# Attention, experts and MLP on one core: the stores of the attention's rows issued by ACT instead of SyncE

## The reference, cut to what matters

```python
# attention: batch 4, heads 8, sequence 576, head size 64
scores = scale * q @ k.T                     # heads 0-3: the last 32 positions; heads 4-7: every 32nd
attn = exp(scores - max); attn /= attn.sum() + 1e-09
x = (attn @ v)                               # -> rows of 2304 tokens x 512
# experts: gate by x @ w_gate (8 experts), rows with x @ w_skip <= 0 pass through
out[sel] = x[sel] + gate * (relu(x[sel] @ w1[e]) @ w2[e])
# then an MLP 512 -> 2048 -> 512 with leaky relu over all rows
```

## Time and profile before

| What | Value |
|---|---|
| median of 3 runs | 760.3 us (759.5 to 762.51) |
| the profiled execution's own time | 757.96 us |
| its span in the trace | 755.9 us |
| busy, of the span | PE 712.7 us (94%), DVE 279.1 (37%), ACT 231.7 (31%), POOL 184.3 (24%) |
| chain that ended last, by engine | PE 86%, DVE 4%, DMA 3%, ACT 3%, issue 3% |
| attention | from the start to the end of the last `xo`, 139.8 us |
| stores `x_rows<-xo`, local (8) | 288.0 KB each, median 7.5 us from issue to landing |

### The profile page before, as it was taken

How to read it: one execution, slowest core, us unless ns; L and a number is a source line. 1 busy time by engine, 2 the same in 40 slices (tenths; PEclk the granted TensorE clock), 3 DMA queues, 4 the chain that set the end, 5 groups by cost and what they waited for, 6 DMA issues and landing times.

```text
span 755.9 us, 12260 instructions
## 1 busy us (share of the span) xinstructions
PE 712.7 (94%) x4674; PEld 662.7 (88%) x4674; DVE 279.1 (37%) x597; ACT 231.7 (31%) x505; POOL 184.3 (24%) x173
## 2 busy tenths in 40 slices
PE   4999999776998999999999999999999999999997
PEld 3899999666998999998999998999999899999996
DVE  5867778458212111113232223223232322323222
ACT  2667666331111111122232223222232322223222
POOL 5242220104197777761100300210030011001000
PEclk9999999896999999999999999999999999999999
DMA  8484845574788989940100200110020001001001
GB/s 174 107 190 114 230 123 158 171 251 124 275 266 285 307 286 310 316 151 20 42 1 1 84 1 0 43 42 1 0 83 0 0 28 55 0 0 43 1 0 42
DMA packets 68653, 81.76 MB, mean 108 GB/s; under 512 B 26137, under 2 KB 47417, under 8 KB 68602
## 3 DMA queue, kind: packets, MB, share of 16 engines
q1 hardware_dynamic: 60040, 58.60, 26.0%
q0 software_dynamic: 7504, 22.44, 9.3%
q10 hardware_dynamic: 1058, 0.02, 0.1%
HBM read 68.84 MB, written 12.21 MB: 107 GB/s over the span
## 4 chain that ended last, share of the span: by engine, by line
PE 86%; DVE 4%; DMA 3%; ACT 3%; issue 3%; SPq 0%; another core or an unknown queue 0%; POOL 0%; ACTq 0%; POOLq 0%; DVEq 0%
PE psum L1679 26%; PE psum L1696 26%; PE psum L1565 9%; PE psum L1581 8%; PE psum L1443 4%; PE psum L1464 3%; ACT kt L884 2%; PE psum L1415 2%; PE psum L1453 2%; PE psum L1434 1%; PE psum L1598 1%; PE psum L1591 1%; DVE sc L1063 1%; DMA x_sb<-x_rows 1%; DMA x_rows<-xo 1%
## 5 line engine op out<-in xcount | busy, mean ns | idle before, releaser
L1380 DVE SCALAR_TENSOR_TENSOR g_act<-g_raw 128x384 f32<-128x384 f32 x96 | 53.6, 558 | 229.4 <-ACT g_raw L1019 229.4
L1679 PE MATMUL psum<-x2h,wih 128*128 128x384 f32 x384 | 130.7, 340 | 1.5 <-issue 1.5
L1679 PE MATMUL psum<-x2h,wil 128*128 128x384 f32 x384 | 129.4, 337 | 0.0
L1679 PE MATMUL psum<-x2l,wih 128*128 128x384 f32 x384 | 128.9, 336 | 0.0
L1019 ACT ACTIVATE g_raw<-psum 128x384 f32<-128x384 f32 x96 | 47.2, 492 | 235.7 <-PE psum L1679 235.7
L1696 PE MATMUL psum<-woh,g_l 128*128 128x512 f32 x288 | 114.0, 396 | 0.0
L1696 PE MATMUL psum<-wol,g_h 128*128 128x512 f32 x288 | 113.7, 395 | 0.0
L1696 PE MATMUL psum<-woh,g_h 128*128 128x512 f32 x288 | 112.2, 390 | 0.5 <-DVE g_l L1384 0.5
L857 POOL DMA_INDIRECT out_dram<-o_sb,idxo x15 | 16.0, 1067 | 282.7 <-ACT o_sb L1014 279.7
L1565 PE MATMUL psum<-xt,wring 128*128 128x160 f32 x512 | 81.6, 305 | 1.5 <-issue 1.5
L1581 PE MATMUL psum<-hp,wring 128*128 128x160 f32 x512 | 78.4, 299 | 1.3 <-issue 0.7
(11 more groups left out here) (210 smaller groups left out, 869.0 us busy)
## 6 DMA issues: line engine op xcount, KB each, us to landing
wring<-in_moe_w_dram SPq DMA_DIRECT2D x64, 512.0 KB
x_sb<-x_rows SPq DMA_DIRECT2D x4, 1024.0 KB, 6.3
stage<-in_moe_w_in_dram POOLq DMA_DIRECT2D x4, 1024.0 KB
stage<-in_moe_w_out_dram POOLq DMA_DIRECT2D x4, 1024.0 KB
q_st<-in_q_dram SPq DMA_DIRECT2D x7, 576.0 KB
k_st<-in_k_dram SPq DMA_DIRECT2D x7, 576.0 KB
vs<-in_v_dram SPq DMA_DIRECT2D x20, 128.0 KB, 8.2
x_rows<-xo SPq DMA_DIRECT2D x8, 288.0 KB, 7.5
```

The lines of the kernel that those rows point to most:

```text
L1380: dve.scalar_tensor_tensor(out=g_act[:, f % 2, :], in0=g_raw[:, f % 2, :], scalar=LEAK, in1=g_raw[:, f % 2, :], op0=ALU.mult, op1=ALU.max) ...
L1679: last = pe.matmul(bank[f % 2][:, 0:MT * P], wt[:, c, f * P:(f + 1) * P], xp[:, T.par, c, :], start=(c == 0 and n == 0), stop=(c == KD - 1 ...
```

## The change

The stores leave SP's list. ACT issues each of them after the exponentials of the group four places on, and the last four after its last `probs_out`. The wait for `s_xo` moves with them. Nothing is computed otherwise, and the DMAs are the same in number, shape and address.

```diff
@@ SP @@
                     sp.wait_ge(s_xo, NG * b + g + 1)
-                    if g in (2, 5) or g >= NL:
-                        x_store(sp, b, g)
                     if b + 1 < B:
                         v_load(sp, b + 1, g)
@@ ACT @@
+            def stored(b, g):
+                if g in (2, 5) or g >= NL:
+                    act.wait_ge(s_xo, NG * b + g + 1)
+                    x_store(act, b, g)
+
...
                     exps(b, g)
+                    if NG * b + g >= 4:
+                        stored(*divmod(NG * b + g - 4, NG))
...
             for g in (NG - 2, NG - 1):
                 probs_out(B - 1, g)
+            for g in range(NG - 4, NG):
+                stored(B - 1, g)
```

## The result

The changed kernel takes 752.16 us (median of 6 runs, 751.3 to 755.44), the kernel before, run beside it, 759.9 us (6 runs, 757.51 to 762.51). The ratio is 0.9909, with a 95% interval of 0.9885 to 0.9934: faster by 0.9%. (Of 759.9 us that is 6.9 us; the two medians by themselves lie 7.7 apart, in six runs each that spread over 4 to 5 us.) The forecast was 755.8 us with a range of 753.3 to 763.0; the time lies 1.1 us under that range. The direction and the mechanism came as forecast; the gain is larger than the sum said. The profiled execution took 751.3 us, with a span of 749.5 (before: 757.96 and 755.9).

The account below looks back on a forecast made before the run. PE was taken to wait at the attention's end for loads of v that SP issues late; -4.6 + 1.1 - 0.3 - 0.7 = -4.5 us, from the 760.3 us median to 755.8 us, range 753.3 to 763.0.

Parts of the forecast that it names:

- What bounds the kernel now: Attention's end, batch 3: PE waits ahead of the last two values products for loads of v that SP issues late.
- the loads of v aren't the cause: Rival: both gaps at the attention's end stay, only ACT's costs remain: +1.1 us, 761.4 us; chance 0.05.
- The end of the attention: Last values products: both gaps go, last xo at 135.2 instead of 139.8 us: -4.6 us, bounds -5.1 and -4.2.
- The stores leave SP: SP's list: 21 stores, 13.8 us, go; last loads of v issued until about 122.4 instead of 136.2 us.
- The stores on ACT inside the pipeline: Three boundaries between batches: stores on ACT delay copies of k that PE awaits: +1.1 us, bounds 0 and +4.8.
- The start of the router: After the last xo: clock stays up, but ACT's stores and zero row come late: -0.3 us, bounds -0.7 and +0.9.
- The last data: Router's fourteenth tile: last store goes out earlier, PE's wait for x_load(3) goes: -0.7 us, bounds -0.7 and 0.
- ACT's stores queue behind SP's issues: Rival: each store on ACT waits half an SP issue, 0.4 us: sum -0.4, 759.9 us; chance 0.19.
- ACT inherits SP's long stalls: Rival: stalls like SP's 2.75 and 3.48 us hit ACT's stores, 4.3 us per boundary: 768.7 us; chance 0.14.
- ACT hides all of it: Rival: no cost at the boundaries and the clock's full gain: -6.5 us, some 754 us; chance 0.10.

Follow-up runs that it names:

- The pair with the delay: 28 unread transposes added to PE's list in batch 0 of both kernels: the kernel before 756.87 us (1.0005), the changed kernel 753.29 us (0.9957).
- SP with its list filled up again: The changed kernel with 21 filler DMAs on SP where stores of batches 0 to 2 had stood: 763.54 us, 1.0087 against the kernel before.

## Why the prediction was wrong in size

*What bounds the kernel now* was right: the gaps are waits for loads that SP issues too late. The pair with the delay shows that SP's list sets the end, and SP with its list filled up again brings the gap back. The rival "the loads of v aren't the cause" falls.

*The end of the attention* is the step that failed, as a term of the sum that was sized too small: "**-4.6 us**", with bounds of -5.1 and -4.2. With the boundaries it said -3.5 us for the last `xo`; the means over three executions say 134.78 - 140.04 = -5.3. Nearly all of the difference of 1.8 us lies in three parts, all readable. I had taken PE's position from one execution, where it reached batch 1 at 45.75; the changed kernel's mean is 44.96: 0.8 us. I had taken SP's from the same one, with the last `xo` at 139.39, where the mean is 140.04: 0.65 us. And the boundaries cost 0.26 us less than the 1.1. My end for PE was good: from 139.39 - 3.5 = 135.9, less 0.8 and 0.26, comes 134.8, which is the measured mean. What failed is that this term is a difference between two chains, PE's and SP's list, and one execution gives one draw of it. The waits of the three executions of before show the same: 4.8 us in the one I used, 7.7 and 5.6 in the others. My bounds held only what the store on ACT could cost, not that the base could move.

*The stores leave SP*: the loads were to be issued by 122.4; it was 127.52, 125.11 and 126.22, in none of the three before 125. The 13.8 us took each store at its usual length and let the excess pass on, and it did pass. But SP's other DMAs grew by more than that excess: 88.5 - 76.6 = 11.9 us against 5.8 (9.4 us in the means of three executions). The sum held the rest of SP's list for fixed. It was without effect here, since the margin was large.

*The stores on ACT inside the pipeline*: "**+1.1 us**" against 3 x 0.28 = 0.84 measured. The mechanism is right to the hundredth at step 1 (0.81 us between the exponential and the copy of k); at step 9 I had allowed 0.05, and there was nothing. The store put ahead of the exponentials takes the whole away, which shows that this is the cost. At the attention's end the copy came 0.50 us later where I had +0.46.

*The start of the router*: "**-0.3 us**" against 0.0 (3.38 us in both kernels). "The clock should stay up" was wrong: it was at its lower level for 3.4 us instead of 6.8 (from windows of the kernel before: 0.59, 0.50, 0.50 and 0.70 between 136 and 144 us). In the other executions, read in the same way, it was 6.8 and 3.4 us in the changed kernel, and 10.2 us in the two others of the kernel before. What I had named as the counterweight, ACT's stores and the zero row, is the bound: with the clock held at 1.00 only 0.17 us are won, with the zero row away as well 0.68.

*The last data*: "**-0.7 us**" against -0.68, -0.90 and -0.92; the wait is gone in all three executions of the changed kernel. That it shortened the whole isn't shown, as the next paragraph says.

Summed anew: -5.3 (with the boundaries) + 0.0 - 0.8 = -6.1 us. The three comparisons gave 0.9909, 0.9912 and 0.9914, that is -6.5 to -6.9 us, with intervals of 1.4 to 2.5 us to either side. The spans of the three profiled executions of each kernel differ by 754.7 - 749.7 = 4.9 us at the mean. The sum lies between; these are three draws each, and whether a microsecond of the gain is elsewhere these runs can't tell. From the last `xo` to the first product of the MLP stage it takes between 198.7 and 201.8 us in the kernel before and between 199.2 and 201.1 in the changed one, with means of 199.9 and 200.2. This stretch holds the wait for `x_sb`, and the 0.8 us saved there can't be seen in it: what the three profiles show of the gain is the 5.3 us at the last `xo`. So the rival that the stores' order at the end makes the gain finds no support there either. Part of the miss against the range is the scale it was measured on: the kernel before had a median of 759.9 to 760.3 us in the first comparison and of 757.05 to 757.49 in the three later ones. The three ratios of the changed kernel, put on the 760.3 us that the forecast started from, give 753.4, 753.6 and 753.8, all just inside the range.

The rivals. *ACT's stores queue behind SP's issues*: not seen on ACT. A store takes 748 ns at the median there, beside an SP that issues with hardly a pause, and 767 ns on SP. The rule of the Trainium skill's page Perfetto Trace Analysis, section "DMA Instruction — HWDGE (DVE, Sync)", that the generator is locked for exclusive use and the wait is inside the duration, would have made them longer; by the measurement, such a wait on ACT is too small to matter here. The one store of 1.355 us is no sign of it: in all nine profiles of kernels that store from ACT, the first strided store that ACT issues takes 1.35 to 1.36 us, whatever SP does beside it, and no other on ACT takes over 0.81. Whether some of the growth of SP's own issues is such a wait stays open; the unchanged median of 751 ns speaks against a wait in every one. *ACT inherits SP's long stalls*: no, they stayed with SP, whose longest load of v went from 3.28 to 4.23 us. I had called both stalled stores "behind loads of q and k"; the one of 3.48 us stands behind three loads of v, one of which took 3.28 itself. ACT's long store costs nothing: the next instruction of ACT starts under it at 45.12, and the one after that waited for PE. *ACT hides all of it*: no, 0.28 us per boundary. Its time of about 754 was nearest to the result, but for another reason.

## What to carry to other kernels

A wait between an engine and an in-order issuer is the difference between two chains, and each of them moves by itself from one execution to the next. Before such a wait is taken as the size of a gain, look at when each chain starts, and ask what the wait would be with the faster chain a microsecond or two earlier; a deliberate delay of known length on one of the two engines (nothing measurable lost, or all 3.07 us) tells which of them sets the time.

A list of issues that was shortened isn't shortened by the length of what was taken out: here stores of 19.6 us left SP's list, and SP was through with it 8.7 us earlier.

A DMA on ACT cost nothing here where the engine waited next anyway, and its issue time less what its predecessor covered (0.28 of 0.77 us) where a copy followed that another engine needed. One place earlier in the code took away all of the cost here: 0.84 us at the boundaries.

When the bound moves, the next one should be priced by its own edit: holding the clock up was worth 0.17 us as long as ACT came late.

## What the runs showed of the chip that I had not expected

A DMA on ACT starts with the instruction ahead of it, and even ahead of one that stands before it in the code if that one isn't started yet: the store at 44.62 us stands behind the exponential of step 10, which starts at 45.12, and behind the copy that starts at 44.63.

The stores land after 4.3 us at the median when ACT issues them and after 7.5 when SP does, among SP's loads. SP's stalls of 2.75 and 3.48 us in a store did not move to ACT with it, but to SP's own next loads (up to 4.23 us). The first strided store from ACT takes 1.35 us, all later ones at most 0.81.

The granted clock fell at the end of the attention in the changed kernel, although PE's idle stretches there are only 0.55 and 1.13 us; with 12 unread transposes, which leave a stretch of 0.26 us ahead of the router, it stayed at 1.00.
